# Output weights loaded behind a later operand load, and their splits moved to match, in a fused retention and feed-forward kernel

## The reference

```python
scores = scale * np.matmul(q, k.transpose(0, 1, 3, 2))
attn = np.matmul(scores * Dmat, v)            # Dmat: lower triangle, powers of gamma
# block 1, d_ff = 2048
h = x @ w_in
g = np.where(h >= 1, h, np.where(h <= -1, 0.0, (h + 1) ** 2 / 4))
x = g @ w_out
# block 2, d_ff = 1536
a = x @ w_a
b = x @ w_b
return (a * b @ w_out2).astype(np.float32)
```

## Time and profile before

| What | Value |
|---|---|
| Median of three runs | 941.91 us |
| Profiled execution, own time | 943.27 us |
| Span of the profiled execution | 941.5 us |
| Mean granted TensorE clock | 0.975 |
| PE busy | 888.4 us (94%) |
| PE weight loads busy | 793.8 us (84%) |
| DVE busy | 480.6 us (51%) |
| ACT busy | 333.9 us (35%) |
| Operand loads `wop<-w_ops` | 36, 1792 KB each, median 7.5 us to landing |
| Output weight loads `wo_raw<-w_out` | 9, 1024 KB each, median 5.8 us to landing |
| DMA over the span | 136.91 MB, mean 145 GB/s |

### The profile page before, as it was taken

One profiled execution on the slowest core, in us unless ns is written; L12 is line 12 of the kernel. 1 busy time (PEld: TensorE's weight loads), 2 busy tenths in 40 slices (PEclk: granted clock), 3 DMA queues, 4 the chain that ended last, 5 costly groups with the idle time before them and its releaser, 6 DMA issues.

```text
span 941.5 us, 13001 instructions
## 1 busy us (share of the span) xinstructions
PE 888.4 (94%) x5232; PEld 793.8 (84%) x5232; DVE 480.6 (51%) x829; ACT 333.9 (35%) x598; POOL 36.9 (4%) x54
## 2 busy tenths in 40 slices
PE   6999999999999999999999979797997979799798
PEld 6998888888998888888899969697997969799796
DVE  4776565555667556656364327443233744333243
ACT  1236554444555445444343323222232422223120
POOL 4640000000000000000000000000000000000000
PEclk9999999999999999999999989899898989989899
DMA  9994000222340333214374253543325554432532
GB/s 347 321 368 166 1 1 1 100 101 101 142 161 21 128 133 122 101 79 157 118 262 180 79 212 145 202 157 141 139 87 224 193 201 157 162 119 106 224 96 68
DMA packets 33453, 136.91 MB, mean 145 GB/s; under 512 B 2673, under 2 KB 13425, under 8 KB 28785
## 3 DMA queue, kind: packets, MB, share of 16 engines
q1 hardware_dynamic: 33248, 135.87, 38.8%
q10 hardware_dynamic: 144, 0.20, 0.1%
HBM read 109.32 MB, written 26.74 MB: 145 GB/s over the span
## 4 chain that ended last, share of the span: by engine, by line
PE 90%; DMA 8%; SPq 1%; issue 0%; DVE 0%; ACT 0%; POOL 0%; POOLq 0%; DVEq 0%; ACTq 0%
DMA wop<-w_ops 7%; PE score_b L518 5%; PE score_b L522 5%; PE score_b L520 5%; PE score_a L518 4%; PE score_a L520 4%; PE score_a L522 4%; PE score_a L472 4%; PE kv_b L489 4%; PE score_a L473 3%; PE score_b L473 3%; PE score_a L474 3%; PE kv_b L491 3%; PE kv_b L490 3%; PE ret_b L491 3%; PE ret_b L490 3%
## 5 line engine op out<-in xcount | busy, mean ns | idle before, releaser
L518 PE MATMUL score_b<-xop_hi,wop 128*128 128x384 f32 x288 | 100.5, 349 | 42.1 <-DMA wop<-w_ops 42.0
L712 DVE TENSOR_TENSOR gate_w<-relu_s,relu_r 128x512 f32<-128x512 f32 (+1 forms) x80 | 51.1, 638 | 96.9 <-ACT relu_r L889 96.8
L522 PE MATMUL score_b<-xop_hi,wop 128*128 128x384 f32 x288 | 99.4, 345 | 0.0
L520 PE MATMUL score_b<-xop_lo,wop 128*128 128x384 f32 x288 | 99.2, 344 | 0.0
L518 PEld LDWEIGHTS score_b<-xop_hi,wop 128*128 128x128 f32 x288 | 55.8, 194 | 46.1 <-issue 44.1
L898 ACT ACTIVATE gh<-gated 128x512 fp32r<-128x512 f32 (+1 forms) x80 | 47.2, 590 | 106.0 <-DVE gated L715 106.0
L518 PE MATMUL score_a<-xop_hi,wop 128*128 128x384 f32 x216 | 77.4, 358 | 0.0
L520 PE MATMUL score_a<-xop_lo,wop 128*128 128x384 f32 x216 | 77.0, 357 | 0.0
L721 DVE TENSOR_TENSOR gl<-gated,gh 128x512 fp32r<-128x512 f32 (+1 forms) x80 | 51.1, 639 | 50.7 <-ACT gh L898 50.6
L522 PE MATMUL score_a<-xop_hi,wop 128*128 128x384 f32 x216 | 76.7, 355 | 0.0
L749 DVE TENSOR_TENSOR a<-score_a,u 128x384 f32<-128x384 f32 x36 | 20.1, 557 | 88.4 <-PE score_a L522 88.4
(11 more groups left out here) (129 smaller groups left out, 2144.9 us busy)
## 6 DMA issues: line engine op xcount, KB each, us to landing
wop<-w_ops SPq DMA_DIRECT2D x36, 1792.0 KB, 7.5
w_ops<-op_hi SPq DMA_DIRECT2D x12, 896.0 KB, 4.6
w_ops<-op_lo SPq DMA_DIRECT2D x12, 896.0 KB, 6.4
kq<-k_q SPq DMA_DIRECT2D x16, 576.0 KB, 6.8
wo_raw<-w_out SPq DMA_DIRECT2D x9, 1024.0 KB, 5.8
kvt<-kv_tok SPq DMA_DIRECT2D x16, 512.0 KB, 6.0
ab_raw<-w_ab SPq DMA_DIRECT2D x12, 512.0 KB, 3.7
w1a_raw<-w SPq DMA_DIRECT2D x10, 512.0 KB, 9.3
```

The costliest lines, as they stand in the source:

```text
L518: pe.matmul(o, w[:, 0, at], xop_hi[b][:, k, :], start=(start and k == 0), stop=False, skip_group_check=True)
L520: pe.matmul(o, w[:, 0, at], xop_lo[b][:, k, :], start=False, stop=False, skip_group_check=True)
L522: mm = pe.matmul(o, w[:, 1, at], xop_hi[b][:, k, :], start=False, stop=(k == 1), skip_group_check=True)
L712: nc.vector.tensor_tensor(gate_w[:, 0:WIDTHS[t]], relu_s[:, 0:WIDTHS[t]], relu_r[:, 0:WIDTHS[t]], ALU.add).then_inc(gatew_ready, 1)
```

## The change

Three things move, and nothing is added or removed. The load of a group's output weights is queued behind `load_ops(4q + 2)`, where it stood behind `load_ops(4q)`. ACT and DVE split tiles 4q and 4q + 1 in step 4q + 2, tile 4q + 2 in step 4q + 3, and tile 4q + 3 in step 4q + 4; step 4q + 1 has no split. The last two of these are the steps in which they were split before. The waits inside `load_out`, `round_out` and `split_out` stay.

```diff
+        def outs_split(step):
+            return {0: [step - 1], 1: [], 2: [step - 2, step - 1], 3: [step - 1]}[step % GROUP] if step else []
...
             for u in range(WBUF, STEPS2):
                 load_ops(u)
-                if u % GROUP == 0 and u >= 2 * GROUP:
+                if u % GROUP == 2 and u >= 2 * GROUP:
                     load_out(u // GROUP)
...
                 add_rows(u, 1)
                 if u < STEPS2:
-                    if 0 < u:
-                        split_out(u - 1)
+                    for v in outs_split(u):
+                        split_out(v)
...
-                elif u == STEPS2:
-                    split_out(u - 1)
+                else:
+                    for v in outs_split(u):
+                        split_out(v)
...
-                    round_out(u - 1)
+                    for v in outs_split(u):
+                        round_out(v)
```

## The result

The changed kernel takes 882.16 us, median of four runs (882.0 to 882.61), beside 942.25 us for the kernel before in the same comparison (941.65 to 944.2). The ratio is 0.936, with a 95% interval of 0.9343 to 0.9376: 60.1 us less. The spans of the two profiled executions, from the first to the last instruction, differ by 941.5 - 880.1 = 61.4 us.

A forecast was written before the change was run, and what follows sets the result against it. PE was taken as the bound, with seven stalls of 8.76 us, 61.3 in all. Taken from 943.27 and 941.91 us, this gave 882.0 and 880.6: predicted 881, own range 878 to 885, 8-in-10 range 877 to 891.

The forecast's parts named there:

- The cause: SP's queue in block 2: operands of step 4q + 1 stood behind an output load waiting for later shares; seven PE waits, 42.0 us.
- The sum: Block 2's groups: 54.48 us with a stall against 45.72 without, 8.76 us each, seven times 61.3 us saved.
- The operands of 4q + 2: Operand load now ahead of the output load: landing bounded by 7.2 to 12.3 us, budget 13.4, so no cost.
- The bound stated for the output weights: Output weights issued near the end of step 4q land in 5.4 to 9.5 us, needed 22.9 us later; no wait added.
- The splits: Step 4q + 2 gains one split on ACT and DVE: cost nothing, at most 10 us in nine groups if uncovered.
- third rival: Restarts behind PE's stalls cheaper than their slow matmuls look: 899.9 us at the extreme, 890.5 with half the clock's part; 3%.
- The clock: PE in block 2: without stalls the granted clock should stay at 1.00.
- the rival of a longer dense stretch: Block 2: clock falls in a dense stretch longer than the 84 us seen, giving back about 21 us: 902 us; 2%.
- The rule of the Trainium skill: All seven PE restarts would cost under 9.4 us, the saving be at most 51.4, the time 891.9; prediction preferred the trace.
- No wait stayed in the first group or behind the stores: Rival: a later wait stays in one or two groups, 8.76 us each: 889.8 us with one, 898.5 with two; 5%.
- The slower case: Rival: PE's wait moves to step 4q + 2; slower from a landing of 19.7 us on, 951 us at 21; 1%.

## Why the prediction was right

The forecast was 881 us, from 882.0 and 880.6; the measured median is 882.16. The mechanism and the size both came out.

- *The cause.* Right. The load moved alone gives 882.33 us, and a queue of its own 882.27. With the load in its old place and the new splits the seven waits are back.
- *The sum.* 61.3 us expected, 61.7 found in block 2, 61.4 between the spans, 60.1 between the medians. In its parts, in block 2: PE's idle time is 42.1 us shorter, where the sum had 42.0 of waits, and its busy time 19.6 us, where the sum had 19.3 for the clock and its surroundings. The matmuls put into the gap show 2.65 us per stall on their own (2.5 was worked out). It is not a constant: 1.8 us for the stall put back (8.1 less 6.3), and some 3.2 us for the one at 822.87. The sum used the mean of five periods, which evens this out. That the total came out within about 1 us is in part luck: the four times of the kernel before alone spread over 2.6 us.
- *The operands of 4q + 2.* Bounded by 7.2 and 12.3 us, taken as up to 9.7, they landed in 7.1 to 7.4. The output load behind them does not slow them; it is slower itself (median 9.6 us, up to 10.5, where it was 5.8 and up to 9.5 in the earlier trace rows). The bound stated for the output weights, 9.5, was 1.0 us short, with 22.9 us to spare.
- *The splits.* The `u2` copy stands 0.52 us later and the next `a0` just fits, as worked out. That they could stay where they were was not said in the prediction; it only costed the move at nothing.
- *A slip.* The third rival's 890.5 us, with half of the clock's part, is 941.9 - 42.0 - 9.65 = 890.3. Nothing hangs on it.
- *The clock.* 1.00 from 461 to 850 us, so the rival of a longer dense stretch is out.
- *The rule of the Trainium skill*, "TensorE: Matmul & The Clock Gate", "Part 1: The HAM clock gate", that ramping up costs under 1% of a typical kernel's span: here the seven restarts cost 19.6 us of PE's busy time in block 2, 2.1% of 941.5 us, and avoiding six of them alone is worth 14.5 us. The measurement decides; the 891.9 us that the prediction took from the rule was 9.7 too high. The section says this of the matmuls at the start of a kernel; that it would also bound seven restarts was the prediction's reading.
- *The rivals.* No wait stayed in the first group or behind the stores. The budget that counted, 13.4 us against 7.3, leaves about 6 us. The slower case needs loads that go out some 7.6 us later than they do.

## What to carry to other kernels

When PE waits for a load, look first at what stood ahead of it in the issuing queue, and what that waited for: a load that needs a late event belongs behind the loads that need only early ones. Price a stall by the period between like points with and without it, not by the wait alone, since the clock behind it adds to it (here 1.8 to 3.2 us on top of some 6). Before moving companion work along with a load, try the load alone; here the moved splits brought margin but no time.

## What the runs showed of the hardware

- Short waits left the clock alone in some cases and not in others. With waits of 1.4 to 1.7 us in every step the window from 560 to 600 us stayed at 1.00, and none of the 26 waits of up to 2.0 us in that run had slow matmuls behind it. All four of 2.3 to 2.7 us had, all three of 3.0 to 3.3 us with the loads held back to p7, and one of 1.9 us behind the needless matmuls.
- Half clock need not begin with the restart. Behind waits of 1.9, 2.4, 2.6 and 3.3 us the first matmuls followed one another at full pace, and the spacing of 0.32 us began 0.4 to 1.7 us after the restart. Who looks only at the first matmul behind a gap (0.41 or 0.66 us) misses it.
- Needless matmuls in a gap made the kernel faster, by 14.5 us of 942.
- Two loads issued in one queue 0.4 us apart landed in order, and the first as if alone (operands in 7.1 to 7.4 us, with 7.2 alone); the second bore the delay (output weights in 9.3 to 10.5 us, where they took 5.4 to 5.9 when they went ahead of the operands).
